# One block per engine with one branch at the end, and a gather issued ahead of the last shared pieces on GpSimd

## The reference

```python
flat = logits.flatten()
order = np.argsort(-flat)
for idx in order:
    tok, e = (int(idx) // E, int(idx) % E)
    if assigned[tok] >= 0 or counts[e] >= cap:
        continue
    assigned[tok] = e
    counts[e] += 1
...
for e in range(E):
    mask = assigned == e
    h = np.maximum(x[mask] @ w1[e], 0.0)
    out[mask] = h @ w2[e]
...
g = x @ w_gate
silu = g * (1.0 / (1.0 + np.exp(-g)))
val = x @ w_val
return (silu * val @ w_out).astype(np.float32)
```

## Time and profile before

| | |
|---|---|
| median of 3 runs | 913.92 us (912.94 to 914.73) |
| the profiled execution, its own time | 914.68 us |
| its span, first to last instruction | 912.9 us |
| PE busy | 853.5 us (94%) |
| DVE, ACT, POOL busy | 512.2, 280.4, 253.2 us |
| mean granted clock of TensorE | 0.966 of full speed |
| attention's block | 0 to about 149 us |
| first expert, with the shared pieces | about 178 to 280 us |
| last store issued | 897 us |

### The profile page before, as it was taken

How to read it: one execution, slowest core, us unless ns; L and a number is a source line. 1 busy time by engine, 2 the same in 40 slices (tenths; PEclk the granted TensorE clock), 3 DMA queues, 4 the chain that set the end, 5 groups by cost and what they waited for, 6 DMA issues and landing times.

```text
span 912.9 us, 17432 instructions
## 1 busy us (share of the span) xinstructions
PE 853.5 (94%) x6582; PEld 801.4 (88%) x6582; DVE 512.2 (56%) x1057; ACT 280.4 (31%) x505; POOL 253.2 (28%) x200
## 2 busy tenths in 40 slices
PE   6999996699969999999999999999999999999991
PEld 4788874399869999999999999999999999999991
DVE  6999985637824464457445634664365536533330
ACT  1344441223214232422332332333233332333210
POOL 2322210165944023403240414050305130522001
PEclk8999997699979999999999999999999999999996
DMA  8789960400310022003200410030013002300000
GB/s 333 267 331 334 337 220 35 153 13 23 100 43 26 0 91 72 27 0 103 60 26 0 129 42 18 20 127 26 17 63 101 17 9 69 95 26 1 1 1 29
DMA packets 25858, 77.27 MB, mean 85 GB/s; under 512 B 3808, under 2 KB 10464, under 8 KB 22880
## 3 DMA queue, kind: packets, MB, share of 16 engines
q1 hardware_dynamic: 22752, 67.39, 21.2%
q0 software_dynamic: 3072, 9.44, 3.3%
HBM read 67.38 MB, written 9.44 MB: 84 GB/s over the span
## 4 chain that ended last, share of the span: by engine, by line
PE 74%; POOL 3%; DVE 2%; issue 1%; DMA 1%; ACT 0%; POOLq 0%; ACTq 0%
PE ps_up L1572 44%; PE ps_acc L1572 26%; PE ps_turn L818 2%; POOL gated_low L1231 2%; POOL w_low L1375 1%; PE ps_turn L1578 1%; PE ps_turn L838 0%; PE ps_turn L823 0%; DVE quick_at_row L794 0%; DMA x_tok<-x_rows,slot_token 0%; DMA x_tok<-x_rows,from_rows 0%; DVE quick_over_cut L740 0%; POOL out L1397 0%; PE ps_up L1578 0%; POOL x_tok L1369 0%
## 5 line engine op out<-in xcount | busy, mean ns | idle before, releaser
L1375 POOL TENSOR_TENSOR w_low<-w_raw,w_high 128x768 fp32r<-128x768 f32 x60 | 130.3, 2178 | 256.3 <-ACT w_high L1463 255.9
L1572 PE MATMUL ps_up<-z_high,gated_high 128*128 128x384 f32 x576 | 197.5, 343 | 0.2 <-DVE z_low L1530 0.2
L1572 PE MATMUL ps_up<-z_high,gated_low 128*128 128x384 f32 x576 | 195.7, 340 | 0.0
L1572 PE MATMUL ps_up<-z_low,gated_high 128*128 128x384 f32 x576 | 194.0, 337 | 0.0
L1572 PEld LDWEIGHTS ps_up<-z_high,gated_high 128*128 128x128 f32 x576 | 108.7, 189 | 0.9 <-issue 0.5
L1572 PEld LDWEIGHTS ps_up<-z_low,gated_high 128*128 128x128 f32 x576 | 108.7, 189 | 0.0
L1572 PEld LDWEIGHTS ps_up<-z_high,gated_low 128*128 128x128 f32 x576 | 108.6, 189 | 0.0
L1535 DVE TENSOR_TENSOR act_out<-ps_up,act_out 128x384 f32<-128x384 f32 x96 | 53.5, 558 | 94.5 <-ACT act_out L1479 92.7
L1482 ACT CAST u_high<-act_out 128x384 fp32r<-128x384 f32 x96 | 49.2, 513 | 170.5 <-DVE act_out L1539 170.5
L1572 PE MATMUL ps_acc<-gated_high,u_high 128*128 128x384 f32 x288 | 97.5, 339 | 1.8 <-DVE u_low L1542 1.8
L1572 PE MATMUL ps_acc<-gated_high,u_low 128*128 128x384 f32 x288 | 96.8, 336 | 0.0
(11 more groups left out here) (164 smaller groups left out, 1433.0 us busy)
## 6 DMA issues: line engine op xcount, KB each, us to landing
w_raw<-in_experts SPq DMA_DIRECT2D x64, 384.0 KB, 3.1
qka_in<-in_qka SPq DMA_DIRECT2D x23, 1026.0 KB, 8.4
gated_raw<-in_gated SPq DMA_DIRECT2D x12, 576.0 KB, 6.6
v_in<-in_v SPq DMA_DIRECT2D x24, 192.0 KB, 8.3
x_rows<-y_rows SPq DMA_DIRECT2D x24, 192.0 KB, 5.0
qka_in<-in_qka SPq DMA_DIRECT2D x1, 512.0 KB, 5.5
out<-o_tok,to_rows POOLq DMA_INDIRECT x24, 2.6
x_tok<-x_rows,from_rows POOLq DMA_INDIRECT x21, 3.2
```

The lines of the kernel that those rows point to most:

```text
L1375: pool.tensor_tensor(w.low[:, m % RING, :], w.raw[:, m % RING, :], w.high[:, m % RING, :].bitcast(F32), ALU.subtract).then_inc(w_low_ready, 1)
L1572: mm = pe.matmul(acc, lhs[a], rhs[b], start=(first and i == 0), stop=(last and i == 2))
```

## The change

There are two parts.

**POOL in the first expert.** The shared pieces wait for the GV four pieces back in place of two. `w_low` of the next expert's first three pieces is written behind shared pieces 4, 5 and 6 in place of 6, 7 and 8. The gather stands ahead of pieces 10 and 11 in place of behind them. `AHEAD` on ACT is as it was.

**One block.** `layers`, `exact_routing` and `layers` again no longer open blocks of their own. Each returns five functions, one per engine, and one block calls them in a row. After the first run each engine waits for the verdict, reads `failed` once and has one branch over all the rest. The last store stands outside any branch. SP waits at the end of its part for the stores to land; before, POOL did.

```diff
-def where_failed(eng, failed):
-    return eng.If(eng.value_load(failed[0:1, 0:1], min_val=0, max_val=1) > 0)
+def has_failed(eng, quick):
+    eng.wait_ge(quick.judged, 1)
+    return eng.value_load(quick.failed[0:1, 0:1], min_val=0, max_val=1)
+
+def meet(eng, sem):
+    eng.drain().then_inc(sem, 1)
+    eng.wait_ge(sem, 5)
...
+            sp.wait_ge(rows_moved, 96 * E - apart)
...
                 if split_gated:
-                    for j in range(GC):
-                        if j >= 2:
-                            pool.wait_ge(v_ready, j - 1)
+                    for j in range(GC - 2):
+                        if j >= 4:
+                            pool.wait_ge(v_ready, j - 3)
                         w.split_gated_low(pool, j)
-                        if 6 <= j < 6 + RING - 1:
-                            split_low(e + 1, j - 6)
+                        if 4 <= j < 4 + RING - 1:
+                            split_low(e + 1, j - 4)
...
                 pool.wait_ge(x_turned, K1 * e + K1)
                 gather(e + 1, 2 * e + 2)
+                if split_gated:
+                    for j in range(GC - 2, GC):
+                        w.split_gated_low(pool, j)
                 split_low(e + 1, RING - 1)
                 pool.wait_ge(rows_moved, 96 * e + 96 - apart)
...
-                    pool.wait_ge(quick.judged, 1)
-                    with pool.If(pool.value_load(failed[0:1, 0:1], min_val=0, max_val=1) < 1):
-                        store(E - 1, 96 * (E - 1) + 48 - apart, 2 * E, one_by_one=False)
-                        pool.wait_ge(rows_moved, 96 * E - apart)
+            store(E - 1, 96 * (E - 1) + 48 - apart, 2 * E, one_by_one=False)
...
+        with nc.Block() as block:
...
+            @block.gpsimd
+            def _(pool):
+                first.gpsimd(pool)
+                with pool.If(has_failed(pool, quick) > 0):
+                    meet(pool, first_done)
+                    exact.gpsimd(pool)
+                    meet(pool, exact_done)
+                    again.gpsimd(pool)
```

More of the change, by code:

```diff
@@ L1 @@
+from collections import namedtuple
 from contextlib import ExitStack
@@ L979, in _ @@
[L979 to L990, removed]
@@ L1075, in phase @@
                 take(p)
[L1077 to L1113, removed]
@@ L1115, in _ @@
-        @block.tensor
-        def _(pe):
+            dve.wait_ge(ready, 8)
+            dve.wait_ge(consts_in, 16 * 7)
+            with dve.Fori(0, PHASES) as p:
+                at[:] = [p * EXACT_LINKS, 0]
+                phase(p)
+                assert at[1] == EXACT_LINKS, at[1]
+            at[:] = [PHASES * EXACT_LINKS, 0]
+            choose()
+            link(dve.tensor_scalar(is_over[:], best[:], -BIG, None, ALU.is_gt))
+            link(dve.tensor_tensor(over[:], choice[:], by_tile(is_over), ALU.mult))
@@ L1237, in chunk, with layers @@
         return of[:, bass.ds(2 * i + r, 1), :].rearrange("p a n -> p (a n)")
-def layers(nc, x_rows, stored, slot_token, order, failed, w, quick, out, again):
+def layers(nc, sems, x_rows, stored, slot_token, order, w, quick, out, again):
     run = "_again" if again else ""
@@ L1320, in layers @@
         quick.use(ps_x)
[L1322 to L1333, removed]
-                        sp.sem_inc(loads_begun, 1)
[L1335 to L1356, removed]
@@ L1358, in _, with sync, expert, ring @@
-        @block.gpsimd
-        def _(pool):
+        def sync(sp):
+            def expert(p):
+                if not again:
+                    sp.wait_ge(quick.order_ready, p + 1)
+                    sp.sem_inc(loads_begun, 1)
+                return sp.value_load(order[0:1, bass.ds(p, 1)], min_val=0, max_val=E - 1)
+            def ring(e, m, p, half):
+                for i in range(RING):
+                    if p is not None:
+                        sp.wait_ge(w_low_ready, FC * p + RING * half + i + 1)
+                        sp.sem_inc(loads_begun, 1)
+                    sp.dma_start(w.raw[:, i, :], w.experts[e, m + i]).then_inc(raw_in[i], 16)
+            e = expert(0)
+            ring(e, 0, None, 0)
+            if not again:
+                sp.wait_ge(first_rows[T3 - 1], 16)
+            ring(e, RING, 0, 0)
+            with sp.Fori(0, E - 1) as p:
+                e = expert(p + 1)
+                ring(e, 0, p, 1)
+                ring(e, RING, p + 1, 0)
+            for i in range(RING):
+                sp.wait_ge(raw_in[i], 16 * 2 * E)
+            sp.wait_ge(rows_moved, 96 * E - apart)
@@ L1491, in expert, with vector @@
                     act.copy(o_tok[:, t, :], ps_acc[t][:, 0:DM]).then_inc(o_copied, 1)
-            with start(act):
-                for m in range(RING):
-                    split_high(0, m)
-                for k in range(K1):
-                    x_part(k, k, ps_acc[k])
-                with act.Fori(0, E - 1) as e:
-                    expert(e)
-                expert(E - 1, last=True)
-        @block.vector
-        def _(dve):
+            for m in range(RING):
+                split_high(0, m)
+            for k in range(K1):
+                x_part(k, k, ps_acc[k])
+            with act.Fori(0, E - 1) as e:
+                expert(e)
+            expert(E - 1, last=True)
+        def vector(dve):
             def x_part(n, k, bank):
```

217 lines of the change are left out of this document (138 added, 79 removed).

## The result

The changed kernel takes 922.32 us (median of 9 runs, 917.25 to 925.67) against 914.24 us before (9 runs): ratio 1.0086, 95% interval 1.0072 to 1.01, so 8 us slower. The forecast was 915.2 us. Its runs are spread over 8.4 us, those of the kernel before over 2.5 us. The profiled execution took 922.32 us itself, with a span of 920.4 us.

The account below looks back on a forecast made before the run. PE was taken as busy nearly all the time, losing 11.6 us in the first expert and 9.7 us in end blocks. +12.3 - 10.7 = +1.6 us on 914.68, against the median 913.92, rounded to 915.2 us; range 911 to 919.5.

Parts of the forecast that it names:

- three waits for shared pieces: First expert: PE idles before GV(5), GV(6), GV(7) through POOL, ACT and DVE: 6.9, 6.6 and 5.1 us, 18.6 in all.
- low clock behind them: First expert: each of the three waits brings one stretch at 1.2 GHz costing 1.9 us, 5.7 us together.
- given back (gather, its low clock, `u_low`): First expert: the gather no longer waits for pieces 10 and 11, returning 8.3 + 1.9 + 1.4 = 11.6 us.
- first expert: First expert: loses 24.3 us in place of 11.6, taken as +12.3 us; bounds +8 to +14.5.
- the end: After the last store: merging blocks and moving branches ends the span at 902.1 instead of 912.8, -10.7 us; bounds -9.6 to -13.
- the pieces behind the gather are covered: First expert: gather and moved pieces 10 and 11 are ready 1 to 2.5 us before PE needs them.
- rival 1: First expert: the three waits stand but the low clock is mostly avoided; -4.3 us, so 911; chance 0.11.
- rival 2: The end: the one long branch needs a code load on POOL or SP, 3.4 to 3.9 us; 918.9 us; chance 0.11.
- rival 3: First expert: the chain through ACT doesn't form, so it gains 11.6 us; 892 us in all; chance 0.03.
- rival 4: The end: nothing gained, because another wait of 10 us takes its place; 926 us; chance 0.03.
- one waits until the other is through: First expert, DVE's L794 beside POOL: 1.72 us alone, 2.57 beside POOL; `w_low` 3.35 in place of 1.81.
- Up to here PE runs as before: First expert, before GV(5): pieces 0 to 4 are ready early, and PE finishes P(3) at 230.7 as before.

Follow-up runs that it names:

- e5_steps_aside: Changed kernel plus two GpSimd waits: shared piece 3 for DVE's fourth over_cut, piece 10 for `u_low` of piece 8; 914.79 us, ratio 1.0015.

## Why the prediction was wrong

Point by point, for the profiled execution:

| term | forecast | measured |
|---|---|---|
| three waits for shared pieces | 6.9 + 6.6 + 5.1 = 18.6 us | 6.4 + 6.1 + 4.8 = 17.3 us |
| low clock behind them | 3 x 1.9 = 5.7 us | 1.8 + 2.1 + 2.8 = 6.7 us |
| given back (gather, its low clock, `u_low`) | 11.6 us | all three are gone: 11.6 us as sized before |
| DVE held up by POOL, with the low clock behind it | none | 2.6 + 1.5 and 2.8 + 1.9 = 8.8 us |
| first expert | +12.3 us | +20.3 us |
| the end | -10.7 us | -10.9 us |

The low clock is what the GVs took beyond the 3.3 us that each takes at the full clock: 5.14, 5.39 and 6.12 us. The measured terms of the first expert add up to 21.2 us, 0.9 more than its 20.3; 0.6 of this is a short wait for `quick_at_row` that is no longer there (5.9 us before, 5.3 after), the rest is open.

**Right.** That three waits would stand in the place of one, where, and by which chain; that they alone cost 24 us (24.3 forecast, 24.0 measured, a closeness that is partly luck, since the waits came out 1.3 us shorter and the low clock 1.0 us dearer); that the pieces behind the gather are covered (PE had no fourth wait for POOL); and the size of the end. There too a part is luck: POOL's drain was to start 0.65 us behind the last issue and take 4.0 us. It started before that issue and took 5.8, and so ended 4.5 us behind the issue, near the 4.7 forecast. Rivals 1 to 4 didn't happen: the clock fell in all three waits, no branch on POOL or SP was long, the chain formed, and the end gained.

**The step that failed** is the one that says of DVE and POOL "one waits until the other is through", and with it "Up to here PE runs as before" and "no fourth wait is counted": waits of PE for DVE were put at nothing. The sum even counts a hold-up of DVE, the 1.4 us for `u_low`, as given back. The rows of L794 showed a DVE instruction that waits for one instruction of POOL, about a microsecond. I took that for the most that could happen, and so didn't ask where the looser waits and the moved pieces would make POOL run without a stop. They do so twice, for 12 and 6 instructions (seven with the `w_low` behind them), and a DVE instruction that came in the middle waited for the rest of the run: over_cut up to 3.0 us beyond its own time, `u_low` 5.6 to 7.0 us. PE had 0.4 us of slack at the first place and about 2.9 us at the second, so 2.6 and 2.8 to 4.1 us reached it. `e5_steps_aside` shows the size: taking both away gives back 7.5 us in the medians, and 9.6 us of the first expert in the profiles, where the table's term is 8.8. The forecast, which lacks this term, is 915.2 us, and that run measured 914.79.

The Trainium skill's page "SBUF — State Buffer", section "SBUF: two separate sides", says that GpSimd and VectorE share a pair of ports, which a VectorE instruction with two inputs in SBUF also needs, and that whoever starts first holds it for the whole instruction. The rows agree that one waits for the other. They go further than one instruction: `u_low` took 6.22 us, while the instructions of POOL in that run took about 1.0 us each and the last 1.79, and here the measurement decides.

The range, 911 to 919.5, was too narrow for the same reason: its bounds came from the clock and the branches, and none from DVE. Some sums of the prediction don't close either: 913.92 + 1.6 is 915.5, not 915.2; rival 1 is priced at 4.3 us, though two low stretches are 3.8; and the bounds of the two terms (+8 to +14.5 and -9.6 to -13) allow 908.9 to 918.8, not 911.5 to 918. None of this reaches the measured 922.3.

## What to carry to other kernels

When work is moved ahead on one engine, ask for each instruction on which other engine's table its input depends; here three `w_low` stood two pieces too early for ACT, and that alone cost 22 us. Waits that space out a helper engine's work can be worth more than they cost (4.5 us with `w_low` early, nothing that the medians show with it late): look for the runs that appear when they are loosened, and for DVE instructions with SBUF inputs that fall into them. Branches over long unused code belong behind the work of an engine that finishes early, not between meetings of all engines.

## What the runs showed of the hardware

- A DVE instruction with its inputs in SBUF that starts in an unbroken run of GpSimd tensor instructions can wait for the end of the run: 4.01 us in place of 0.99, 6.15 to 7.55 us in place of 0.56. It doesn't always: in two of three profiles of one program over_cut was through after 1.1 us. A wait on a semaphore between GpSimd's instructions that is not yet met lets it in (1.08 and 1.27 us in `e5_steps_aside`).
- GpSimd's drain behind indirect transfers took 4.0 us when it started 1.8 us after the last issue had ended, with all of them landed, and 5.6 to 6.5 us in the profiles with one block, where it started before or with the last issue; it then ended 4.5 to 5.2 us after that issue.
- PE's taken branch took 3.4 to 3.9 us over long bodies and 0.2 us over one empty instruction. Packets on the queues named "instruction" appear beside the long ones (seven behind 903 us before) and none beside the short ones.
